# One attention slot per MLP step, one PSUM bank for both up products, and a new order of first loads

## The reference

```python
for t in range(S):
    kt, vt, rt, wt = (k[:, :, t], v[:, :, t], r[:, :, t], w[:, :, t])
    cur = np.einsum('bhd,bhe->bhde', u[None] * kt, vt)
    y[:, :, t] = np.einsum('bhd,bhde->bhe', rt, state + cur)
    state = wt[:, :, :, None] * state + np.einsum('bhd,bhe->bhde', kt, vt)
...
x = (x @ w_a) * (x @ w_b) @ w_out            # d_model 384, d_ff 1536
h = x @ w_in2                                # d_ff 2048
return (np.maximum(h, 0) + alpha * np.minimum(h, 0)) @ w_out2
```

## Time and profile before

| | |
|---|---|
| median of 3 runs | 1099.53 us (1099.34 to 1099.66) |
| the profiled execution | 1099.37 us, its span 1097.6 us |
| PE busy | 1032.8 us, 94% |
| DVE, ACT, POOL busy | 521.7, 303.7, 207.5 us |
| TensorE clock granted, mean | 0.995 of full speed |
| start to first gated matmul | 82.9 us |
| one tile with attention in it (tile 2) | 77.0 us |
| one tile without (tile 7) | 56.3 us |

### The profile page before, as it was taken

How to read it: one execution, slowest core, us unless ns; L and a number is a source line. 1 busy time by engine, 2 the same in 40 slices (tenths; PEclk the granted TensorE clock), 3 DMA queues, 4 the chain that set the end, 5 groups by cost and what they waited for, 6 DMA issues and landing times. The chain is left out here.

```text
span 1097.6 us, 28888 instructions
## 1 busy us (share of the span) xinstructions
PE 1032.8 (94%) x12448; PEld 996.9 (91%) x12448; DVE 521.7 (48%) x1017; ACT 303.7 (28%) x611; POOL 207.5 (19%) x167
## 2 busy tenths in 40 slices
PE   2658999999999999999999999999999999999998
PEld 2548889899898998998998999999999999999998
DVE  4565374263363454453542222555555555455554
ACT  2223523323323322323232243322121221222121
POOL 4545453123122222221330041400000000000000
PEclk9999999999999999999999999999999999999999
DMA  6241540221211311401200131301001010101000
GB/s 172 85 131 45 161 126 24 82 63 49 68 51 48 89 52 28 117 23 54 78 24 13 33 97 63 102 1 44 23 21 44 1 43 0 43 0 44 1 22 22
DMA packets 45688, 60.09 MB, mean 55 GB/s; under 512 B 4097, under 2 KB 45569, under 8 KB 45569
## 3 DMA queue, kind: packets, MB, share of 16 engines
q1 hardware_dynamic: 44240, 58.21, 17.8%
q10 hardware_dynamic: 1328, 0.13, 0.1%
HBM read 44.17 MB, written 14.16 MB: 53 GB/s over the span
## 5 line engine op out<-in xcount | busy, mean ns | idle before, releaser
L799 DVE TENSOR_TENSOR g_sb<-a_g,b_ps 128x384 f32<-128x384 f32 x96 | 53.2, 554 | 274.0 <-PE b_ps L137 220.7
L934 DVE TENSOR_SCALAR leaky_low<-leaky_h_ps,leaky_al 128x384 f32<-128x384 f32 x128 | 79.0, 617 | 177.7 <-PE leaky_h_ps L137 171.1
L886 ACT ACTIVATE leaky_g_hi<-leaky_g_sb 128x384 fp32r<-128x384 f32 x128 | 67.2, 525 | 296.6 <-PE leaky_acc L137 225.9
L365 POOL TENSOR_TENSOR r_in<-r_in,f_y 112x384 f32<-112x384 f32 x80 | 92.5, 1169 | 193.4 <-PE products L577 192.8
L135 PE MATMUL acc<-g_hi,weights_hi 128*128 128x384 f32 x288 | 104.5, 363 | 0.3 <-DVE g_lo L805 0.3
L135 PE MATMUL a_ps<-x_hi,weights_hi 128*128 128x384 f32 x288 | 101.5, 352 | 3.3 <-DVE x_lo L129 3.3
L409 ACT ACTIVATE a_g<-a_ps 128x384 f32<-128x384 f32 x96 | 47.2, 492 | 196.3 <-PE a_ps L137 196.3
L409 ACT ACTIVATE g_hi<-g_sb 128x384 fp32r<-128x384 f32 x96 | 50.4, 525 | 173.0 <-DVE g_sb L799 173.0
L137 PE MATMUL acc<-g_hi,weights_lo 128*128 128x384 f32 x288 | 97.6, 339 | 0.0
L136 PE MATMUL acc<-g_lo,weights_hi 128*128 128x384 f32 x288 | 97.4, 338 | 0.0
L137 PE MATMUL a_ps<-x_hi,weights_lo 128*128 128x384 f32 x288 | 97.2, 338 | 0.0
(11 more groups left out here) (75 smaller groups left out, 2229.4 us busy)
## 6 DMA issues: line engine op xcount, KB each, us to landing
x_in<-y_dram SPq DMA_DIRECT2D x16, 576.0 KB, 4.7
k_in<-in_k_dram SPq DMA_DIRECT2D x16, 336.0 KB, 3.5
r_in<-in_r_dram SPq DMA_DIRECT2D x16, 336.0 KB, 4.3
w_v<-in_w_dram SPq DMA_DIRECT2D x16, 336.0 KB, 3.2
stage<-in_w_out_dram SPq DMA_DIRECT2D x14, 384.0 KB, 3.2
w_v<-in_v_dram SPq DMA_DIRECT2D x16, 288.0 KB, 3.1
y_dram<-f_y SPq DMA_DIRECT2D x32, 144.0 KB, 2.8
y_dram<-x_in SPq DMA_DIRECT2D x8, 576.0 KB, 3.0
```

The lines of the kernel that those rows point to most:

```text
L365: pool.tensor_tensor(halves(t, h, 1), halves(t, h, 1), decay(j, h, 0), ALU.mult).then_inc(r_stepped[j], 1)
L799: dve.tensor_tensor(g_sb[:, :], a_g[:, :], b_ps[:, 0:TT], ALU.mult).then_inc(g_ready, 1)
L886: return act.activation(out_, in_, ACT.Copy)
L934: dve.tensor_scalar(low[f % 2][:, :], h, 0.0, al[:, f:f + 1], ALU.min, ALU.mult).then_inc(low_ready, 1)
```

## The change

1. PSUM: `products` has five banks. Four belong to the attention: levels use banks 0 and 1 or 2 and 3 in turn (`level_bank`), all else banks 2j and 2j + 1 (`stream_bank`). The fifth takes a, and b too if the steps on both sides have a slot (`b_ps(g)`); otherwise b takes a bank of the attention that is free. `up` is cut into `up_a` and `up_b`. `up_b` waits for the copy of a of its own step. `up_a` waits for the multiply of the step before, where that b lay in the fifth bank.
2. PE's order is a(g), down(g-1), b(g), then the slot, in a step behind a slot; and a(g), b(g), down(g-1), then the slot, in a step that has none ahead. The slot takes the phase of both streams. Phase 7 now is the key-values of stream 0, phase 8 those of stream 1, phase 9 the outputs of both.
3. Outputs: stream 1 puts its heads in swapped rows (`hd ^ j`), and the state products of both streams alternate.
4. DVE: `step_k` of stream 0 stands ahead of `g_lo`; all else, the whole of phase 0 among it, behind. `carry_states` moves with its key-values. ACT: some copies move behind the copy of a (`attend_late`), and the weight splits ahead of `g_hi`.
5. SP: in phase 9 the R load of stream 1, the stores of both streams, then both W loads.
6. Start: masks are loaded first, `ident` last and waited for in phase 6 alone; a tiny copy loads ACT's table early; the first `step_k` of duo 0 is on DVE; weight pieces are split behind phases 5 to 9 (`EARLY_AT`) instead of 1, 3, 5, 7 and 9.

```diff
-EARLY_AT = [1, 3, 5, 7, 9]
+EARLY_AT = [5, 6, 7, 8, 9]
-FIXED_LOADS = 6
+FIXED_LOADS = 4
...
-            products = bank("products", 3)
-            a_ps, b_ps, acc = bank("a_ps"), bank("b_ps"), [bank(f"acc{m}") for m in range(KT)]
+            products, acc = bank("products", 5), [bank(f"acc{m}") for m in range(KT)]
+            a_ps = products[:, 4 * BANK:4 * BANK + TT]
...
-            def bank_of(n, use, side):
-
-                return BANK * ((26 * n + 2 * use + side) % 3)
+            def level_bank(phase, hd):
+
+                return BANK * (2 * ((phase - 1) % 2) + hd)
+
+            def stream_bank(j, side):
+
+                return BANK * (2 * j + side)
+
+            def b_ps(g):
+
+                before, behind = g > 0 and step_at(g - 1) is not None, step_at(g) is not None
+                at = BANK * ((4 if behind else 0) if before else 1 + (g + 1) % 2)
+                return products[:, at:at + TT]
...
                 def load_w(n, j):
                     if n > 0:
-                        sp.wait_ge(products_done[j], after(n - 1, 8))
+                        sp.wait_ge(products_done[j], after(n - 1, 9))
...
-                    elif phase == 8:
+                    elif phase == 9:
+                        if n + 1 < DUOS:
+                            load_r(n + 1, 1)
+                        store_y(n, 0)
+                        store_y(n, 1)
                         if n + 1 < DUOS:
                             load_w(n + 1, 0)
-                            load_r(n + 1, 1)
-                        store_y(n, 0)
-                    elif phase == 9:
-                        if n + 1 < DUOS:
                             load_w(n + 1, 1)
-                        store_y(n, 1)
...
+                def state_products(n, crossed):
+
+                    last = [None, None]
+                    for c in range(CH):
+                        for j in range(2):
+                            for hd in range(2):
+                                par = 1 - hd if crossed else hd
+                                b = 2 * HALF * (n % 2) + 2 * (c % HALF) + par
+                                if b > 0:
+                                    last[j] = pe.matmul(view(products, stream_bank(j, par) + BLOCK * c, [[1, BLOCK]], D, 64 * (hd ^ j)),
...
+                def up_a(g):
                     tile, f = divmod(g, F1)
                     if f == 0:
                         pe.wait_ge(shared.x_ready, tile + 1)
...
+                    pe.wait_ge(a_copied, g)
+                    if g > 1 and step_at(g - 2) is not None and step_at(g - 1) is not None:
+                        pe.wait_ge(g_ready, g)
+                    up(g, "w_a", a_ps, a_done)
+
+                def up_b(g):
+                    pe.wait_ge(a_copied, g + 1)
+                    pe.wait_ge(g_ready, from0(g - 1))
...
+                    up(g, "w_b", b_ps(g), b_done)
...
                 for g in range(TILES * F1):
-                    up(g)
-                    if step_at(g) is not None:
-                        attend_first(step_at(g))
-                    if g > 0:
+                    slot_before = g > 0 and step_at(g - 1) is not None
+                    up_a(g)
+                    if slot_before:
+                        down(g - 1)
+                    up_b(g)
+                    if g > 0 and not slot_before:
                         down(g - 1)
                     if step_at(g) is not None:
-                        attend_second(step_at(g))
+                        pe.wait_ge(g_ready, g)
+                        attend(step_at(g))
...
@@ dve @@
-                    step = step_at(g - 1) if g > 0 else None
-                    if step is not None and not 1 <= step % PHASES <= 4:
-                        attend(step, 1)
...
-                    if step is not None and step % PHASES < 5:
-                        attend(step, 0)
+                    if step is not None:
+                        attend_early(step)
                     dve.wait_ge(g_hi_ready, g + 1)
...
-                    if step is not None and step % PHASES >= 5:
-                        attend(step, 0)
-                    if step is not None and 1 <= step % PHASES <= 4:
-                        attend(step, 1)
+                    if step is not None:
+                        attend(step)
```

More of the change, by code:

```diff
@@ L155, in merges, with copies @@
     return 12 * duo + (0 if phase == 0 else 2 * phase + 2) + part + 1
-def copies(duo, use, side):
-    return 10 * duo + COPIED.index(use) * 2 + side + 1
+def copies(duo, what, j, side):
+    return 10 * duo + (0 if what == "level" else 2 + 2 * j if what == "keys" else 6 + 2 * j) + side + 1
 def states_after(duo):
@@ L381, in attend @@
                     n, phase = divmod(step, PHASES)
[L382 removed]
+                    if phase == 0 and n > 0:
                         first_step_k(n, j)
@@ L504, in _ @@
                     tile, f = divmod(g, F1)
-                    if g > 0 and step_at(g - 1) is not None:
-                        attend(step_at(g - 1), 1)
                     act.wait_ge(a_done, g + 1)
                     act.wait_ge(g_ready, g)
-                    copy(a_g[:, :], a_ps[:, 0:TT]).then_inc(a_copied, 1)
+                    copy(a_g[:, :], a_ps).then_inc(a_copied, 1)
+                    if g > 0 and step_at(g - 1) is not None:
+                        attend_late(step_at(g - 1))
+                    if tile == 0:
+                        for piece in new_pieces(f):
+                            shared.split_hi(act, piece)
                     act.wait_ge(g_ready, g + 1)
@@ L581, in turn_keys @@
                 def turn_keys(n, j):
-                    bank_free(n, 7 + j)
+                    if j == 0:
+                        pe.wait_ge(copied, copies(n, "level", 0, 1))
+                    else:
+                        pe.wait_ge(merged, merges(n, 4, 1))
                     pe.wait_ge(k_last[j], n + 1)
@@ L642, in attend_first, with outputs, attend @@
+                def outputs(n):
+                    for j in range(2):
+                        weighted_values(n, j)
+                    for j in range(2):
+                        pe.wait_ge(r_stepped[j], 6 * n + 6)
+                    state_products(n, False)
+                    for j in range(2):
+                        pe.wait_ge(products_done[j], after(n, 8))
+                    state_products(n, True)
+                def attend(step):
                     n, phase = divmod(step, PHASES)
@@ L786, in _ @@
                 for step in range(BEFORE_TILES):
-                    for j in range(2):
-                        attend(step, j)
+                    attend_early(step)
+                    attend(step)
                 shared.split_x_lo(dve, 0, 0)
```

225 lines of the change are left out of this document (112 added, 113 removed).

## The result

| | before | after |
|---|---|---|
| median of the runs, us | 1099.43 (1099.07 to 1099.66, 4 runs) | 1137.76 (1136.84 to 1138.86, 4 runs) |
| profiled execution, us | 1099.37, span 1097.6 | 1138.04, span 1136.2 |
| first gated matmul, us | 82.90 | 74.67 |
| tile 7 of the gated MLP, first a matmul of its first and of its twelfth step, us | 626.52 to 678.00 | 656.32 to 718.07 |

The ratio is 1.0349 with a 95% interval of 1.0331 to 1.0367. The forecast was 1112.4 us, range 1083 to 1128: the direction was right, the size was not, and the time lies outside the range.

The account below looks back on a forecast made before the run. TensorE's queued work bounds the MLP tiles, latency the start. Start -12, attention visits -7.1, state products -10.9, key-values wait -10.2, shared bank +25.2, late multiply +28 sum to +13.0: 1099.4 becomes 1112.4 us, range 1083 to 1128.

Follow-up runs that it names:

- both edits: The changed kernel without up_b's wait on a_copied where no slot is ahead, and with W loads ahead of the y stores: 1081.91 us, ratio 0.9842.

## What to carry to other kernels

A wait that no one needs is worth looking for right after a change of buffers: here one wait, stated for all steps and needed in some, took 31.8 us. Where an operation moves on a DMA queue or on POOL, ask what it will run beside, since in the MLP a load that landed late cost next to nothing by itself, and moving it back gave 25.6 us, through the engine that it sets going. And price a place of the code where it stands in the program, with what each engine does just there, not by the cleanest instance of it. A long row of short matmuls also has to be fed: this one used up 256 instructions in 1.8 us where the next block took 3.1 to 3.5 us from the start of the one before.

## What the hardware showed beyond the forecast

- PE's supply of instructions can run out: in a row of 192 matmuls 14 to 16 ns apart, with as many weight loads, PE stopped for 1.0 to 2.0 us at the same three positions of its program in all nine kernels that sent the row at full speed. It went on 1.0 to 1.7 us behind the end of the 16 KB packet that brings the next 256 instructions; where that packet had ended earlier, or the row went by in 2.96 us instead of 1.8, there was no stop. With 1.35 us more of work in the row one of the stops was gone and the two others were less than half as long.
- VectorE's products with two SBUF inputs took 4.64 us beside POOL and 1.3 without, a factor of 3.5, though each single POOL step lasts 1.0 to 1.5 us only.
- The same short stop has two prices. With W loaded first, PE stopped 1.2 us ahead of f = 9 in tiles 1, 2, 4 and 5. In the kernel with that edit alone the granted clock fell to the lower level (1.2 GHz) behind three of them (f = 9 took 7.98 us), behind one it stayed (6.44). With both edits the same stops (f = 8 of 7.68 us) were followed by a fall in tile 4 alone. What tells them apart wasn't tried.
